# Paused sends, finer landing marks, reordered first loads, and a first stage in 15 chunks of 120-token tiles

## The reference, cut to what matters

```
w = softmax(weight, axis=-1)                 # 8 heads x 7 taps
out[b,s,h,:] = sum_k w[h,k] * x_pad[b, s+k, h, :]        # causal, 6 zeros in front
x = out.reshape(14336, 192)
# mixture 1: each token goes to the one expert with the largest logit
logits = x @ w_gate;  e = argmax(logits);  gate_w = softmax(logits)[e]
x = gate_w * (relu(x @ w1[e]) @ w2[e])       # w1: 192x1024, w2: 1024x192, 8 experts
# mixture 2: noisy logits, the two best experts, their softmax weights
noisy = x @ w_gate + log1p(exp(x @ w_noise)) * noise
out = sum over the two best experts of weight * (relu(x @ w1[e]) @ w2[e])
```

## Time and profile before

| what | value |
|---|---|
| time before (median of 3 runs) | 1995.59 us (1994.42 to 1995.81) |
| the profiled execution's own time | 1985.47 us |
| its span | 1983.5 us |
| PE busy | 1886.2 us (95%) |
| POOL busy | 929.5 us (47%) |
| VectorE (DVE) busy | 1274.3 us (64%) |
| ScalarE (ACT) busy | 914.4 us (46%) |

### The profile page before, as it was taken

One profiled execution on the slowest core, in us unless ns is written; L12 is line 12 of the kernel. 1 busy time (PEld: TensorE's weight loads), 2 busy tenths in 40 slices (PEclk: granted clock), 3 DMA queues, 4 the chain that ended last, 5 costly groups with the idle time before them and its releaser, 6 DMA issues.

```text
span 1983.5 us, 50949 instructions
## 1 busy us (share of the span) xinstructions
PE 1886.2 (95%) x14103; PEld 1832.6 (92%) x14104; DVE 1274.3 (64%) x4251; ACT 914.4 (46%) x2425; POOL 929.5 (47%) x1301
## 2 busy tenths in 40 slices
PE   7986689999999999799999999999999999999998
PEld 5666689999999999799999999999999999999998
DVE  4675378787887788755555655655655655655555
ACT  4553145455555555434444444444444444445444
POOL 3777734343334333444444444444444444444444
PEclk9997799999999999999999999999999999999999
DMA  6644232332332323232231221322322322222221
GB/s 215 233 149 136 79 108 86 116 120 84 113 101 93 117 87 109 81 97 63 64 99 61 66 92 61 100 66 63 101 63 67 97 61 65 96 62 87 78 62 48
DMA packets 114007, 185.92 MB, mean 94 GB/s; under 512 B 21580, under 2 KB 89924, under 8 KB 111808
## 3 DMA queue, kind: packets, MB, share of 16 engines
q1 hardware_dynamic: 73392, 104.86, 17.5%
q0 software_dynamic: 40320, 79.90, 11.9%
q10 hardware_dynamic: 272, 0.92, 0.1%
HBM read 112.10 MB, written 77.61 MB: 96 GB/s over the span
## 4 chain that ended last, share of the span: by engine, by line
PE 83%; DVE 5%; issue 5%; POOL 4%; another core or an unknown queue 1%; DMA 1%; DVEq 1%; ACT 1%; ACTq 0%; SPq 0%; POOLq 0%
PE bank L1145 26%; PE bank L1146 12%; PE bank L1126 8%; PE bank L1129 8%; PE bank L1128 8%; PE bank L1130 8%; PE bank L1127 7%; POOL rows_of_mixture L1229 3%; PE bank L1115 2%; PE bank L996 2%; DVE h_l L843 1%; PE bank L1063 1%; PE bank L1116 1%; POOL pause L1231 1%
## 5 line engine op out<-in xcount | busy, mean ns | idle before, releaser
L1145 PE MATMUL bank<-w2hl,h_h 128*128 128x384 f32 (+1 forms) x2832 | 867.9, 371 | 10.5 <-DVE w2hl L669 3.6
L1146 PE MATMUL bank<-w2hl,h_l 128*128 128x192 f32 (+1 forms) x2832 | 722.9, 255 | 0.0
L843 DVE SCALAR_TENSOR_TENSOR h_l<-bank,h_h 128x512 fp32r<-128x512 f32 x708 | 477.9, 689 | 177.6 <-ACT h_h L557 90.7
L557 ACT ACTIVATE h_h<-bank 128x512 fp32r<-128x512 f32 x708 | 422.4, 597 | 357.4 <-PE bank L1130 316.0
L1145 PEld LDWEIGHTS bank<-w2hl,h_h 128*128 128x128 f32 x2832 | 536.1, 189 | 17.2 <-issue 10.0
L1146 PEld LDWEIGHTS bank<-w2hl,h_l 128*128 128x128 f32 x2832 | 545.1, 192 | 0.0
L1126 PE MATMUL bank<-x_h,w1mh 128*128 128x256 f32 x1416 | 403.4, 285 | 16.9 <-issue 8.9
L1256 POOL DMA_INDIRECT rows_of_mixture<-x_in,pos x248 | 245.9, 992 | 363.3 <-DVE h_l L843 173.3
L1128 PE MATMUL bank<-x_h,w1ml 128*128 128x256 f32 x1416 | 401.0, 283 | 2.2 <-issue 2.2
L1129 PE MATMUL bank<-x_h,w1lh 128*128 128x256 f32 x1416 | 401.8, 284 | 0.8 <-issue 0.8
L1130 PE MATMUL bank<-x_h,w1ll 128*128 128x256 f32 x1416 | 400.0, 282 | 1.1 <-issue 1.1
(11 more groups left out here) (193 smaller groups left out, 1895.9 us busy)
## 6 DMA issues: line engine op xcount, KB each, us to landing
rows<-rows_of_mixture SPq DMA_DIRECT2D x179, 208.0 KB
raw<-in_w_of_both SPq DMA_DIRECT2D x17, 1024.0 KB
raw<-in_w_of_both SPq DMA_DIRECT2D x17, 768.0 KB
x_in<-in_x SPq DMA_DIRECT2D x16, 768.0 KB
out<-zeros SPq DMA_DIRECT2D x61, 192.0 KB
raw<-in_moe_w_turned SPq DMA_DIRECT2D x8, 768.0 KB
rows_of_mixture<-pad_rows SPq DMA_DIRECT2D x21, 208.0 KB, 10.2
rows_of_mixture<-x_in,pos POOLq DMA_INDIRECT x248
```

The source lines that it names most:

```text
L557: nc.scalar.activation(h_h[:, 2 * p:2 * p + 2, :].rearrange("p c t -> p (c t)"), bank[1 + p][:], ACT.Relu).then_inc(hh_ready[m], 1)
L843: V.scalar_tensor_tensor(h_l[:, 2 * p:2 * p + 2, :].rearrange("p c t -> p (c t)"), bank[1 + p][:], 0.0, h_h[:, 2 * p:2 * p + 2, :].rearran ...
L1145: T.matmul(dst, h_h[:, c, tok], both, start=(c == 0), stop=False)
L1146: last = T.matmul(bank[5 + a][:, 0:width], h_l[:, c, tok], w2hl[:, c, 0:width], start=False, stop=(c == F // P - 1))
```

## The change

The first stage gets tiles of 120 tokens, 30 to a sequence (3600 places for 3584 tokens: the first 16 places of each sequence are empty), so 120 tiles in 15 chunks. The empty places are cleared from the counts, and their rows are sent to a spare place of the table. The steps that were tied to chunk numbers (folds, first weights) move up by one chunk. `landed` is counted up in the middle of the next chunk (after its fourth send) where it was after its eighth, and the rows of expert 0 are noted at each of the chunks 4 to 13, with a last column that repeats that of 13. In mixture 1, POOL clears `pause` and waits for it after each of the first three sends of a slot. The noise moves from ScalarE's queue to SP's, behind chunk 1, which moves ahead of the small gates. The subtraction of the largest tap becomes the bias of the exponential, and the band is built head by head. TensorE runs 26 products of 128x128 by 128x512 (bf16) at the start, whose results nobody reads.

```
-TILE = 112
+TILE = 120
+PER_BATCH = -(-SEQ // TILE)
+EMPTY = PER_BATCH * TILE - SEQ
+TILES = BATCH * PER_BATCH
+CHUNKS = TILES // CHUNK
+WARM = 26
-EARLY_AT = [XROW + 2 * k for k in range(4)]
+EARLY_AT = list(range(4, CHUNKS - 1))
+DUE_COLUMNS = len(EARLY_AT) + 1
+MARK_AT = 3
+def empty_tiles(c):
+    return [b * PER_BATCH - c * CHUNK for b in range(BATCH) if c == b * PER_BATCH // CHUNK]
...
             load_chunk(0)
             sp_.dma_start(g1_in..., gate1).then_inc(gates_in, 16)
+            load_chunk(1)
+            sp_.dma_start(noise_in[:], ...).then_inc(noise_loaded, 16)
             for i, g in enumerate((gate2, gate_noise)):
...
-            for c in range(1, XIN):
+            for c in range(2, XIN):
...
-            for half in range(2):
-                act.wait_ge(band_shifted, half + 1)
-                nc.scalar.activation(band[:, heads], band[:, heads], ACT.Exp).then_inc(band_exped, 1)
+            act.wait_ge(band_shifted, 1)
+            act.wait_ge(band_loaded, 16)
+            for h in range(HEADS):
+                nc.scalar.activation(band[:, h], band[:, h], ACT.Exp, bias=tap_low[:, h:h + 1]).then_inc(band_exped, 1)
...
-                link(V.tensor_tensor(band_w[:, heads], keep..., tap_div..., ALU.mult))
-                V.tensor_tensor(band[:, heads], band[:, heads], band_w[:, heads], ALU.mult).then_inc(band_ready, 1)
+            for h in range(HEADS):
+                dve.wait_ge(band_exped, h + 1)
+                V.scalar_tensor_tensor(band[:, h], band[:, h], tap_div[:, h:h + 1], keep[:], ALU.mult, ALU.mult).then_inc(band_ready, 1)
...
+                for t in empty_tiles(c):
+                    link(V.memset(seen_in[0:EMPTY, :, t + 1:t + 2], 0.0))
...
+                    if c == EARLY_AT[-1]:
+                        link(V.tensor_copy(first_count[:, k + 1:k + 2], bank[2][0:1, RANKS:RANKS + 1]))
...
+                for t in empty_tiles(c):
+                    link(last)
+                    last = V.tensor_copy(c_pos[0:EMPTY, c % XROW, t:t + 1], nowhere_i[0:EMPTY])
...
-                V.tensor_scalar(due[:], slots_in[:], -2.0, float(CHUNKS), ALU.mult, ALU.add).then_inc(due_ready, 1)
+                V.tensor_scalar(due[:], slots_in[:], -1.0, float(CHUNKS), ALU.mult, ALU.add).then_inc(due_ready, 1)
...
+            def warm_up():
+                pe.wait_ge(setup_pool, 1)
+                for i in range(WARM):
+                    T.matmul(bank[7][:].rearrange("p (k c) -> p k c", k=4), ones_b[:], bc(ones_b[:].unsqueeze(1), [P, 4, P]),
+                             start=(i == 0), stop=(i == WARM - 1))
...
                     link(G.memset(pause[:], 0.0))
-                if c > 0:
-                    mark_landed(c - 1)
+                    if t == MARK_AT and c > 0:
+                        mark_landed(c - 1)
...
                         G.indirect_dma_start(rows_dram[1], ..., row[:, r, a, :], ...).then_inc(scattered2[r % 2], 16)
+                        if (k, a) != (1, 1):
+                            G.memset(pause[:], 0.0).then_inc(paused, 1)
+                            until((paused, s * 3 + (CHUNKS * CHUNK + 2 * k + a + 1)))
```

More of the change, by code:

```diff
@@ L117, in attention_and_two_mixtures @@
         tap_div = sb("tap_div", [P, HEADS])
-        band_w, band = sb("band_w", [P, HEADS, TILE]), sb("band", [P, HEADS, TILE])
+        tap_low = sb("tap_low", [P, HEADS])
+        band = sb("band", [P, HEADS, TILE])
         g1_in = sb("g1_in", [P, 3, LANES])
@@ L640, in _ @@
             V.tensor_tensor(tap_s[:], tap_in[:], bc(tap_max[:].unsqueeze(2), [P, HEADS, TAPS]), ALU.subtract).then_inc(tap_shifted, 1)
[L641 to L644, removed]
-                V.tensor_tensor(band[:, heads], band[:, heads], bc(tap_max[:, heads].unsqueeze(2), some), ALU.subtract).then_inc(band_shifted, 1)
+            V.tensor_scalar(tap_low[:], tap_max[:], -1.0, None, ALU.mult).then_inc(band_shifted, 1)
             dve.wait_ge(tap_exped, 1)
@@ L650, in _ @@
             dve.wait_ge(masks_ready, 1)
-            for half, heads in enumerate(halves):
-                link(V.tensor_tensor(band_w[:, heads], bc(keep[:].unsqueeze(1), some), bc(tap_div[:, heads].unsqueeze(2), some), ALU.mult))
-                dve.wait_ge(band_exped, half + 1)
-                V.tensor_tensor(band[:, heads], band[:, heads], band_w[:, heads], ALU.mult).then_inc(band_ready, 1)
+            for h in range(HEADS):
+                dve.wait_ge(band_exped, h + 1)
+                V.scalar_tensor_tensor(band[:, h], band[:, h], tap_div[:, h:h + 1], keep[:], ALU.mult, ALU.mult).then_inc(band_ready, 1)
             dve.wait_ge(setup_pool, 2)
@@ L678, in _, with steps_of @@
             C_STEPS = 11
+            def steps_of(c):
+                return C_STEPS + (c == EARLY_AT[-1]) + 2 * len(empty_tiles(c))
             full = [TILE, CHUNK, E]
@@ L755, in _ @@
             for c in range(1, CHUNKS):
-                link = Steps(dve, dve_c, C_STEPS * c)
+                link = Steps(dve, dve_c, sum(steps_of(k) for k in range(c)))
                 choose_first(c, link)
@@ L1339 @@
         if name == "x":
-            padded = np.zeros((BATCH, HALO + SEQ + P, D), a.dtype)
-            padded[:, HALO:HALO + SEQ] = a
-            tiles = np.stack([padded[:, t * TILE:t * TILE + P] for t in range(SEQ // TILE)], 1)
+            padded = np.zeros((BATCH, EMPTY + HALO + SEQ + P, D), a.dtype)
+            padded[:, EMPTY + HALO:EMPTY + HALO + SEQ] = a
+            tiles = np.stack([padded[:, t * TILE:t * TILE + P] for t in range(PER_BATCH)], 1)
             a = np.ascontiguousarray(tiles.reshape(CHUNKS, CHUNK, P, D).transpose(0, 2, 1, 3).reshape(CHUNKS, P, CHUNK * D))
         if name == "moe2_noise":
-            a = np.ascontiguousarray(a.reshape(TILES, TILE, E).transpose(1, 0, 2).reshape(TILE, TILES * E))
+            whole = np.zeros((BATCH, EMPTY + SEQ, E), a.dtype)
+            whole[:, EMPTY:] = a.reshape(BATCH, SEQ, E)
+            a = np.ascontiguousarray(whole.reshape(TILES, TILE, E).transpose(1, 0, 2).reshape(TILE, TILES * E))
         if name == "weight_turned":
```

39 lines of the change are left out of this document (20 added, 19 removed).

## The result

The changed kernel takes 1964.88 us (median of 4 runs, 1964.21 to 1966.47); the kernel before took 1995.7 us beside it (4 runs, 1994.42 to 1997.65). The ratio is 0.9846 (95% interval 0.9834 to 0.9858), 30.8 us faster. The forecast was 1974.5 us with a range down to 1967.0: right in sign, too small by 9.6 us, and the result lies 2 us outside the range.

The account below looks back on a forecast made before the run. POOL's sends were taken to bound the front, TensorE's work the rest after 300 us. Profiled 1985.5 - 6.8 (start to slot 5) - 14.3 (stall) = 1964.4; from the median, 1995.6 - 21.1 = 1974.5 us, range 1967 to 1990.

Parts of the forecast that it names:

- the stall: Hole at 240 to 254 us while POOL sends mixture 1's backlog back to back; 14.3 us, all taken as removed.
- Part 1, the start: Earlier chunk 0 load and faster work after the 26 products: first send 8.2 us earlier, at 24.4 (bounds 4 to 10.5).
- Part 2, 15 chunks: First stage's sends: 962 ns each, 12.49 us a chunk, fifteen 187.3; last landing at 211.7 us, 18.8 earlier.
- The 0.8 us for the mark: POOL's time for the landing mark in each first-stage chunk, counted beside eight sends of 1.45 us; kept in the forecast.
- Part 3, finer marks: Slot 4 waits for all 15 chunks, starting at 215.5; slot 5 at 227.5, gain 6.8; due at 14, slot 4 7 sooner.
- Part 4, paused sends: Mixture 1's backlog sends spaced 1.45 us instead of 1.31 remove 14.3 us (bounds 0 to 14.3); slot 7 at 248.2.
- the argument from the first stage: First-stage sends, with the same pause, ran beside slots 0 to 3 without a hole, so pauses remove all 14.3 us.
- The change to mixture 2: Last eight sends of mixture 1 stand back to back; effect of the pauses taken as 0, bounds -3 (gain) and +2.
- A: Rival: the stall stays, hanging on the branch or number of sends; gain only 6.8, 1988.8 us; chance 0.20.
- D: Rival: earlier chunks move nothing, the front is paced by something thought hidden, the stall moves elsewhere; 1995.6 us; chance 0.05.
- B: Rival: the start is no earlier, held by the 26 products or the loads; 1982.7 us; chance 0.10.
- C: Rival: pauses hold VectorE in every slot of mixture 1, up to 40 us slower; 2014.5 us; chance 0.05.

Follow-up runs that it names:

- pauses alone: The kernel before with only the pauses between mixture 1's sends added: 1970.72 us (ratio 0.9931) on chip B, 1969.64 us (1.001) on chip E.
- after, 112 tokens: The changed kernel with 16 chunks of 112-token tiles again, mark still in mid-chunk: 1979.1 us (ratio 0.9965) on chip C, 1953.6 us (0.993) on chip E.
- after, due at 14: The changed kernel with expert 0's rows noted at chunk 14 too, replacing the repeated column: 1956.91 us (ratio 0.9859) on chip B, 1954.91 us (0.9932) on E.
- one-pause version: The changed kernel with one pause per slot of mixture 1, after the second of its four sends: 1965.5 us, ratio 0.9893, on chip C.

## Why the prediction was wrong

The kernel times side by side (us, medians; a blank was not run):

| chip | before | pauses alone | after | after, 112 tokens | after, due at 14 |
|---|---|---|---|---|---|
| A | 1995.7 | | 1964.9 | | |
| B | 1985.7 | 1970.7 | | | 1956.9 |
| C | 1986.0 | | 1962.3 | 1979.1 | |
| D | 1967.8 | | | | |
| E | 1968.1 | 1969.6 | 1960.5 | 1953.6 | 1954.9 |

The kernels whose sends keep 1.5 us or more apart in the mean agree within 4.4 us wherever they ran; those with quicker sends (before in mixture 1's backlog, the 112-token version in the first stage) move by 25 to 28 us from chip to chip. The traces part the chips in the same way. None of the eight traces of D and E names "remote" between 20 and 300 us. Each of the ten others does, the spaced kernels too: ScalarE and VectorE together 33.5 us in the kernel after on A and 7.5 on C, 44.6 in the pauses alone on B, 68.4 in the kernel before on B, 126.7 in the 112-token version on C. So with spaced sends the hold-up is shorter and falls where TensorE waits anyway; it doesn't end.

**The step that failed** is the one sentence under the sum: "The median is 10.1 us above that execution; the steps are the same size there". The term that was mis-sized is the stall. The sum took 14.3 us for it, and taking it out alone gained 15.0 on chip B. On chip A the change gained 30.8 us; less the 7.7 (5 to 9 by its interval) that it gains on chip E, where nothing stalls, 23 us are left for the stall. On chip C it is 23.7 - 7.7 = 16.0, on chip E it is nothing.

The 10.1 us that were moved along as a constant are a difference between two levels of the same kernel. The profile before fits the level of chips B and C: from slot 63 to the end (mixture 2) it takes 1132.3 us, as the unchanged kernel does on chip B (1132.3), where the kernel after takes 1136.4 on A and 1132.7 on C. From C to A the kernel before is 9.7 us longer and the kernel after 2.6. So of the distance about 2.6 us lie on both kernels (the slower mixture 2 is the likely place), and the change removed 7.1, most likely more of the stall. For chip A this is worked out and not seen: there is no trace of the kernel before at 1995 us. The range had been made from the bounds of the terms in one execution; no end of it said that a removed stall can be longer in the timed runs than in the profiled one.

**The sum's agreement is luck in part.** Between the two profiles the start up to slot 5 gains 6.7 us (forecast 6.8) and slots 5 to 7 gain 14.0 (14.3). But then 2.1 are gained from slot 7 to 60 and 2.6 from 60 to 63, both taken as nothing ("From slot 7 on the program is the same", "I take 0"), and mixture 2 loses 4.0, which the kernel after doesn't lose on C or E. These three cancel to 0.7. On chip C, beside a kernel before of the profile's level, the gain was 23.7 and not 21.1.

**Part 1, the start.** First send at 25.87 us for the forecast 24.4 (bounds 22.1 to 28.6): a gain of 6.7 us, not 8.2. Chunk 0 landed at 9.81 and not at 8.1 to 9: 1.8 us earlier than before instead of at least 2.6, and its matmuls were waiting for it (9.85, idle 1.34 until that DMA). The products end at 8.51 and not at 10. The products alone are worth 5.1 us at the first send and 4.3 in the time, and the order of loads 8.0 at the first send (33.89 for 25.91): each needs the other, and the sum of their single worths is not the gain. The kernel that runs the products with the old loads is no faster than the kernel before.

**Part 2, 15 chunks.** The end came out (212.27 for 211.7) by errors of opposite sign: the first send was 1.5 us late and the 15 chunks took 186.4 us for 187.3. In these there are two more. A send of 120 rows takes longer than one of 128 (line's statistics: ns min, median, max):

```profile
L1253 POOL DMA_INDIRECT rows_of_mixture<-x_row,c_pos x120: 1001/1001/1357, 25.9 to 209.5; - x120
```

The line between 947 and 977 gave 962, and 1001 lies outside both bounds; with its idle time a send takes 1.525 us, and 8 take 12.2. The 0.8 us for the mark, on the other hand, went to nothing, since the mark in mid-chunk waits for sends that ended long before and no gap is left. I had kept the 0.8 and argued only that the mark does not block. The two runs that move the mark alone put its place at 0.44 and 0.6 us a chunk.

**Part 3, finer marks.** Right: slot 4 waits for all 15 chunks (loaded at 213.18, with TensorE idle 23.32 us in front of its transpose, where 30 or more were forecast; on chip E, without "remote" waits, it is 34.94), slot 5 starts at 227.65 for 227.5. Noting chunk 14 as well gives 5.6 us on chip E, measured side by side, where the prediction's remark had said 7: slot 4 starts 7 us sooner, slot 5 only 6.

**Part 4, paused sends.** Slots 5 to 7 take 21.0 us (forecast 20.7), slot 7 starts at 248.66 (248.2). That the pauses remove the hole is shown on chip B both ways (pauses put in: 15.0 us gained; taken out of the changed kernel: the hole is back), and the one-pause version gives part of it. A pause is a cleared tile, a wait and a gap in one; that the gap does it rests on the 112-token version, which has every pause, lacks the gap at the chunk's end, and starts slot 0 at 181.6 us on chip C, where the kernel before, with the same tiles, a later first send and the gap, starts it at 151.7 on chip B. The spacing of 1.45 us was wrong, it is 2.25, and this mattered: 1.44 us without a break holds the engines up on chip C. So the argument from the first stage (that it "had the same pause and ran beside slots 0 to 3 without a hole") stood on the 0.8 us gap at each chunk's end, and it was true only of long holes: in the same profile ScalarE's line 557 waits 6.3 us for "remote" from 150 to 215 us.

**The change to mixture 2**, taken as 0: from slot 60 to 63 the unchanged kernel takes 38.0 us on chip B and 33.9 with the pauses, a gain of 4.1 there; in the profiled pair it is 36.2 and 33.6. The bound of 3 was short. In the body of mixture 1 (slots 7 to 60) all kernels that descend from the changed one take 542.9 to 543.7 us and all that descend from the one before 545.3 to 545.9, on every chip and with or without pauses, products, old loads and late marks. These some 2.4 us were not forecast, and their cause stays open.

**Rivals.** A and D are out by the time alone. B's mechanism is out (the first send is 6.7 us earlier). C (the pauses hold VectorE) is out: the slots of mixture 1 got no longer (543.6 us from slot 7 to 60 for 545.7), and the row that answers to the earlier trace rows keeps its spread with POOL's pauses beside it.

```profile
L857 DVE SCALAR_TENSOR_TENSOR h_l<-bank,h_h x708: 675/691/694, 147.2 to 1950.1; 128x512 fp32r<-128x512 f32 x177
```

The instruction fetch rule of the Trainium skill (Runtime: NRT & Kernel Launch, section Instruction fetch mechanics) would have put the stall at the branch. Against it stand the pauses alone, which leave the branches as they are and take the hole out (15.0 us on chip B), and the DMA records of the kernel before: no packet of an instruction queue starts between 208.8 and 257.0 us, and the engines run again at 253.97. The 112-token version is held up on chip C in the first stage, far from any change of expert.

**What stays open.** Why the chips differ, and what is held up. The profile names it "remote", TensorE shows it as "issue", and POOL itself runs on. The Trainium skill (DMA: Bandwidth & Descriptors, section Latency and other measured facts) names contention for the ports behind the descriptor rings of GpSimd's DMAs as its best guess for why two of the DMA engines are usually slower; it says nothing of compute engines, and no run here shows whether the two have to do with each other. It was not tried whether the same chip keeps its length of stall at another time, so the chips' difference could be one of the time or the place in memory too. The mark in mid-chunk was not run on a chip that stalls, and the unchanged kernel was timed but not traced on D and E.

## What to carry to other kernels

When the timed median lies well above the profiled execution, ask whether the profile is of the same level as the timed runs, and which term of the sum could be the difference: here a stall was 14 us in the profile and, as worked out, about 23 in the timed runs. Indirect sends of GpSimd held up all compute engines on three of five chips: 11 to 15 in a row at 1.3 us, or a whole stage at 1.44 us without a break, cost 9 to 17 us; at 1.53 us in the mean there were still waits, but they fell where TensorE was idle anyway. So leave gaps between such sends (a cleared tile with a wait) as insurance, and judge such a change on more than one chip. The version of this kernel to keep is the one with slot 4 due at 14 chunks: 1956.9 and 1954.9 us on two kinds of chip, while the 112-token version is 1.3 us faster on one and 17 us slower than the changed kernel on the other.

## What the runs showed of the hardware that I had not expected

- The same program (16 chunks of 112 tokens) takes 1979.1 us on one chip and 1953.6 on another, and the kernel before takes 1967.8 to 1995.7 on five (each chip at one time).
- While POOL's sends hold the engines up, TensorE's matmuls go on one by one, 0.7 to 2.1 us apart, and show "issue"; ScalarE and VectorE show "remote".
- An indirect send of 120 rows takes 1.00 us; 112 rows take 0.95 and 128 rows, of another source tile, 0.98.
- TensorE kept its full speed over 1.34 us of idle time at the start (eight matmuls in 1.56 us) and had lost it after 3.30 us (2.92 us).
- POOL's pause leaves 1.02 us idle ahead of the next send where the count it waits for is computed in mixture 1's loop, and 0.30 where it is a constant in the first stage. Which difference of the two places makes it was not tried.
